# Second head's results in the other partition half, and a new order of ScalarE's copies, in a fused recurrence and expert kernel on one Trainium2 core

## What is computed

```python
for t in range(S):
    kt, vt, rt, wt = (k[:, :, t], v[:, :, t], r[:, :, t], w[:, :, t])
    cur = np.einsum('bhd,bhe->bhde', u[None] * kt, vt)
    y[:, :, t] = np.einsum('bhd,bhde->bhe', rt, state + cur)
    state = wt[:, :, :, None] * state + np.einsum('bhd,bhe->bhde', kt, vt)
```

## Time and profile before

| | |
|---|---|
| median of 3 runs | 529.81 us |
| the profiled execution, its own time | 532.97 us |
| its span | 531.0 us |
| TensorE matmul busy | 486.4 us, 92% |
| TensorE weight loads busy | 431.3 us, 81% |
| VectorE busy | 333.4 us, 63% |
| ScalarE busy | 334.9 us, 63% |

### The profile page before, as it was taken

The page is one execution under the profiler, slowest core; times in us unless marked ns, Lnnn a source line. Parts: engine busy times, 40 slices in busy tenths (PEclk is TensorE's granted clock), DMA queues, the critical chain, the costliest instruction groups (busy, mean ns, idle before and its releaser), DMA issues.

```text
span 531.0 us, 18119 instructions
## 1 busy us (share of the span) xinstructions
PE 486.4 (92%) x7516; PEld 431.3 (81%) x7516; DVE 333.4 (63%) x583; ACT 334.9 (63%) x689; POOL 13.7 (3%) x21
## 2 busy tenths in 40 slices
PE   5878999798999897888888899999999999999996
PEld 3667877687878786776434599999999999999996
DVE  8789787788888888642521575555555555555552
ACT  4788796768796977452221575656566656566653
POOL 9100000000000000000000000000000000000000
PEclk9999999899999998999999999999999999999999
DMA  8785585666363615675999220101010101010101
GB/s 166 137 175 120 121 182 105 143 126 115 65 120 67 119 33 167 204 240 156 376 394 373 88 72 1 46 1 46 0 47 1 44 0 45 0 44 1 46 0 44
DMA packets 129385, 56.19 MB, mean 106 GB/s; under 512 B 103328, under 2 KB 128928, under 8 KB 128928
## 3 DMA queue, kind: packets, MB, share of 16 engines
q1 hardware_dynamic: 126112, 54.53, 39.1%
q10 hardware_dynamic: 3200, 0.59, 0.6%
HBM read 50.38 MB, written 4.72 MB: 104 GB/s over the span
## 4 chain that ended last, share of the span: by engine, by line
PE 74%; ACT 10%; issue 6%; SPq 4%; DVE 3%; DMA 2%; ACTq 1%; DVEq 0%
PE bank L758 13%; PE bank L759 13%; PE bank L760 13%; PE lbank L482 5%; PE ybank L526 5%; PE tbank L433 5%; PE bank L748 4%; PE ybank L542 4%; ACT wide L855 4%; PE lbank L509 3%; SPq L374 2%; PE lbank L493 2%; PE ybank L463 2%; DMA w_hi<-in_moe_w_dram 2%; ACT wl L796 1%
## 5 line engine op out<-in xcount | busy, mean ns | idle before, releaser
L758 PE MATMUL bank<-wo_high,h_high 128*128 128x384 f32 x384 | 128.8, 335 | 1.4 <-DVE h_low L1251 1.2
L759 PE MATMUL bank<-wo_low,h_high 128*128 128x384 f32 x384 | 128.4, 334 | 0.0
L760 PE MATMUL bank<-wo_high,h_low 128*128 128x384 f32 x384 | 128.4, 334 | 0.0
L997 ACT ACTIVATE h_relu<-bank 128x384 f32<-128x384 f32 x128 | 62.9, 492 | 72.7 <-PE bank L748 72.4
L1249 DVE CAST h_high<-h_sq 128x384 fp32r<-128x384 f32 x128 | 46.0, 359 | 95.1 <-PE bank L760 86.3
L1085 DVE TENSOR_TENSOR rk<-rk,wl 112x768 f32<-112x768 f32 x80 | 76.5, 957 | 35.4 <-PE lbank L482 17.7
L1251 DVE TENSOR_TENSOR h_low<-h_sq,h_high 128x384 fp32r<-128x384 f32 x128 | 71.5, 558 | 4.5
L758 PEld LDWEIGHTS bank<-wo_high,h_high 128*128 128x128 f32 x384 | 72.1, 188 | 2.6 <-issue 2.2
L759 PEld LDWEIGHTS bank<-wo_low,h_high 128*128 128x128 f32 x384 | 72.1, 188 | 0.0
L760 PEld LDWEIGHTS bank<-wo_high,h_low 128*128 128x128 f32 x384 | 72.1, 188 | 0.0
L1001 ACT ACTIVATE h_sq<-h_relu 128x384 f32<-128x384 f32 x128 | 67.4, 527 | 4.1
(11 more groups left out here) (127 smaller groups left out, 543.2 us busy)
## 6 DMA issues: line engine op xcount, KB each, us to landing
w_sb<-in_moe_w_dram SPq DMA_DIRECT2D x32, 384.0 KB, 4.1
w_hi<-in_moe_w_dram SPq DMA_DIRECT2D x16, 384.0 KB, 9.2
v_tok<-in_v_dram SPq DMA_DIRECT2D x32, 144.0 KB, 3.0
w_lo<-in_moe_w_dram SPq DMA_DIRECT2D x1, 4608.0 KB, 16.5
out_dram<-o_sb SPq DMA_DIRECT2D x8, 576.0 KB, 3.0
nat<-in_r_dram SPq DMA_DIRECT2D x62, 72.0 KB, 2.5
nat<-in_k_dram SPq DMA_DIRECT2D x62, 72.0 KB, 2.7
nat<-in_w_dram SPq DMA_DIRECT2D x60, 72.0 KB, 2.6
```

The source lines that it names most:

```text
L758: nc.tensor.matmul(acc, hi, wo_high[:, fb, :], start=(fb == 0), stop=False)
L759: nc.tensor.matmul(acc, hi, wo_low[:, fb, :], start=False, stop=False)
L760: last = nc.tensor.matmul(acc, lo, wo_high[:, fb, :], start=False, stop=(fb == NF - 1))
L997: nc.scalar.activation(h_relu[fb % 2][:], h_bank[fb % 2][:, 0:GT * P], ACT.Relu).then_inc(relu_done, 1)
```

## The change

The output of `y_near` and `y_far` for head `h` of the pair goes to partition half `par ^ h`. Head 1's tokens then lie in `ybank` with the two halves exchanged, and `y_to_x` copies them back in two copies of 64 partitions, so that it has three copies instead of two. `Y_OUT` is 3 wherever `y_evac` is counted. In ScalarE's order `spread_w` of both pairs goes ahead of `y_to_x(rd - 1, 0)`, and `y_to_x(rd - 1, 1)`, which stood behind `top_level_out(rd, 0)`, goes into the next round, behind `k_out` of pair 0 (for the last but one round: between the two `k_out` behind the loop).

```diff
+    Y_OUT = 3
...
@@ after_attention, k_times_v, y_near and the wait ahead of turn_x @@
-                    pe.wait_ge(y_evac[1], 2 * rd)
+                    pe.wait_ge(y_evac[1], Y_OUT * rd)
...
+            def y_rows(par, h):
+                half = par ^ h
+                return slice(C * half, C * half + C)
+
@@ y_near @@
-                            last = nc.tensor.matmul(ybank[rows, at:at + D], aa[rd % 2][s][rows, PER * h + i, :],
+                            last = nc.tensor.matmul(ybank[y_rows(par, h), at:at + D], aa[rd % 2][s][rows, PER * h + i, :],
@@ y_far @@
-                            rows = slice(C * par, C * par + C)
-                            last = nc.tensor.matmul(ybank[rows, at:at + D], rk[rd % 3][s][a:b, 0, C * c:C * c + C],
+                            last = nc.tensor.matmul(ybank[y_rows(par, h), at:at + D], rk[rd % 3][s][a:b, 0, C * c:C * c + C],
@@ y_to_x @@
-                for h in range(2):
-                    src = ybank[:, 512 * h:512 * h + PER * D].rearrange("p (i n) -> p i n", n=D)
+                for h, a, b, to in ((0, 0, P, 0), (1, C, P, 0), (1, 0, C, C)):
+                    src = ybank[a:b, 512 * h:512 * h + PER * D].rearrange("p (i n) -> p i n", n=D)
                     at = s * PW + h * D
-                    nc.scalar.activation(X[:, :, rd, at:at + D], src, ACT.Copy).then_inc(y_evac[s], 1)
+                    nc.scalar.activation(X[to:to + b - a, :, rd, at:at + D], src, ACT.Copy).then_inc(y_evac[s], 1)
@@ ScalarE's order @@
                 if late:
                     k_out(rd - 1, 0)
+                    if rd > 1:
+                        y_to_x(rd - 2, 1)
                     widen(rd, 1, 1)
                     k_out(rd - 1, 1)
...
                 next_out(5, 1)
+                for s in range(2):
+                    spread_w(rd, s)
                 if late:
                     y_to_x(rd - 1, 0)
                 next_out(6, 1)
-                for s in range(2):
-                    spread_w(rd, s)
                 next_out(7, 2)
                 next_out(9, 1)
                 top_level_out(rd, 0)
-                if late:
-                    y_to_x(rd - 1, 1)
                 next_out(10, 2)
                 top_level_out(rd, 1)
                 if ahead:
                     widen(rd + 1, 0, 1)
-            for s in range(2):
-                k_out(ROUNDS - 1, s)
+            k_out(ROUNDS - 1, 0)
+            y_to_x(ROUNDS - 2, 1)
+            k_out(ROUNDS - 1, 1)
```

More of the change, by code:

```diff
@@ L252, in after_attention @@
             for s in range(2):
-                eng.wait_ge(y_evac[s], 2 * ROUNDS)
+                eng.wait_ge(y_evac[s], Y_OUT * ROUNDS)
         def xt_view(n):
@@ L360, in _ @@
                 for s in range(2):
-                    sp.wait_ge(y_evac[s], 2 * ROUNDS)
+                    sp.wait_ge(y_evac[s], Y_OUT * ROUNDS)
                 sp.dma_start(debug, X[:].rearrange("p a b c -> p (a b c)")).then_inc(stored[0], 16)
@@ L519, in y_near @@
                 else:
-                    pe.wait_ge(y_evac[0], 2 * (rd + 1))
+                    pe.wait_ge(y_evac[0], Y_OUT * (rd + 1))
                 for i in range(PER):
@@ L608, in _ @@
                 pe.wait_ge(top_out[s], 2 * ROUNDS)
-                pe.wait_ge(y_evac[s], 2 * (ROUNDS - 1))
+                pe.wait_ge(y_evac[s], Y_OUT * (ROUNDS - 1))
             turn_x(0, 4)
```

## The result

The changed kernel is slower: 534.48 us median (530.73 to 536.81, 20 runs) against 531.50 us (528.22 to 537.59, 20 runs) before, a ratio of 1.0063 (95% interval 1.0041 to 1.0085), some 3 us. I had forecast 3.6 us less. The page of one execution of the changed kernel, which happened to be the fastest of its 20 runs (530.73 us), shows the shares.

A forecast was written before the change was run, and what follows sets the result against it. A TensorE and a ScalarE stretch bound each round: rounds 2 to 6 -1.5, round 1 -1.1, round 7 -0.8, behind the rounds -0.2, together -3.6 us from 529.8 to 526.2 us, range 520.5 to 535.5.

The forecast's parts named there:

- Two stretches bound a round: TensorE bounds 14.1 us, level 3 of pair 0 to level 5 of pair 1; ScalarE the other 11.5 us.
- Near results at 17 ns, 0.8 us a call: `y_near` in four quarters loads weights at `L509`'s 17 ns: 0.8 us a call instead of 1.5, 0.7 us less.
- rival 1: Near results get no faster, by the row-group rule or the shared bank: +5.7 us, 535.5 us; chance 0.15.
- 0.43 us of the first call arrive: Behind the first `y_near`, level 3 of pair 1 needs `widen`, so only 0.43 of the 0.7 us passes.
- `y_far`'s order at nothing: `y_far` uses four quarters before and after; exchanging the order of two costs nothing, 0.1 us a call either way.
- `spread_w` and the third copy of pair 0 together at nothing, margin 0.2 us: `spread_w`, 1.17 us, fits ScalarE's 1.43 us idle before `y_to_x(rd-1, 0)`, paying for its third copy; else up to 0.3 us a round.
- The copies in their new place, +0.8 us: Pair 1's three `y_to_x` copies, 0.95 us mid ScalarE stretch, less 0.15 us of wait, lengthen it by 0.8 (0.45 to 0.95).
- The sum over rounds 2 to 6, -0.3 each: TensorE stretch -1.1 us plus ScalarE stretch +0.8 us gives -0.3 us a round, -1.5 us in all.
- Round 1, -1.1: The first round has the faster near results but no moved copies yet: -1.1 us.
- The last round -0.8 and what lies behind it -0.2: Round 7: -1.3 on TensorE, +0.5 for copies; behind: two `y_near` calls -1.4, `turn_x` +0.6, last copies +0.3, `x_out` +0.3.
- Rival 4: ScalarE's copies hold more than they last, some 0.3 us a round: -1.8 us in all, 528 us; chance 0.1.
- The base: The sum is taken from the median of three runs, 529.8 us, not from the profiled execution's 532.97 us.

The follow-up runs named there:

- VectorE's copies: Changed kernel with VectorE copying head 1, ScalarE only head 0, `y_to_x` of pair 1 back in its own round; ratio 1.0024 to the kernel before.
- the four quiet profiles: Kernel before and changed kernel, each run twice with all w1 loads behind the recurrence: 559.98 and 560.96 us before, 564.53 and 564.02 us changed.

## Why the prediction was wrong

Point by point, in its own order:

- *Two stretches bound a round.* Right. Every version moved as the stretch in which it changed something, and the chain of the changed kernel runs through the same pieces. (That more than half of TensorE's busy time lies behind 300 us was a misreading: it is 225 of 486 us. Nothing hung on it.)
- *Near results at 17 ns, 0.8 us a call.* Right: 17 ns, and the shared bank did not matter. So rival 1 has fallen: the order of row halves stayed the same, and going round four quarters instead of two nearly halved the spacing. The rule of the Trainium skill that loads overlap matmuls only of another row group ("TensorE: Matmul & The Clock Gate", Part 3, What overlaps and what doesn't), by which there was to be no gain, is not borne out by this trace.
- *0.43 us of the first call arrive.* It was 0.33, for the 0.15 us between `widen` and the matmul behind it.
- *`y_far`'s order at nothing.* Right, 22 to 23 ns.
- *`spread_w` and the third copy of pair 0 together at nothing, margin 0.2 us.* **This step failed.** Two things in it were wrong. The move of `spread_w` cannot pay for input copy 6: on ScalarE's list copy 6 stands directly behind `y_to_x(rd - 1, 0)` before the change as after it, and `spread_w` stood behind copy 6. And the three copies take 1.27 us, not 0.95. So copy 6 came 0.69 us later behind the first copy, turn 8 waited, and a round lost 0.36 us of the near gain; -1.1 us became -0.66. With copy 6 first, turn 8 no longer waited.
- *The copies in their new place, +0.8 us.* 0.86, within its bounds, but in part by luck: the copies cost 1.17 us where I had 0.95, and 0.3 us came back where I had 0.15.
- *The sum over rounds 2 to 6, -0.3 each.* Follows from the above: +0.2 each, +1.0 in all in place of -1.5.
- *Round 1, -1.1.* Its TensorE stretch, from level 3 of pair 0 to the end of level 5 of pair 1, has no issue gap in the four quiet profiles. It takes 14.07 and 14.10 us before, and 13.44 and 13.91 changed: -0.6 and -0.2.
- *The last round -0.8 and what lies behind it -0.2.* Wrong by more than the rounds. From the first `y_near` of the last round to that behind the rounds, where I had -0.8 and +0.6 for the first `turn_x`, the quiet pairs have +1.3 and +1.4 us. The waits that I had priced came out about as forecast (0.8 us ahead at the last `turn_k`, then 0.74 us of waiting where I had 0.6). What I had no term for are issue gaps and the clock, which took the rest. From that `y_near` to the expert part I had -0.8, and it is -0.1 us in both pairs: the two calls give 1.3 us, but `x_out` behind three copies takes 0.7 of it back and the wait for the last copies 0.56 (1.44 us in place of 0.88), where I had 0.3 for each. That is again the length of three copies.
- *Rival 4* (copies that hold more than they last) named the right part, but I gave it 0.1 and a size that still left a gain.
- *The base.* I started from 529.8 us, the median of three runs; that of 20 is 531.5. This is 1.7 of the 8.3 us between forecast and measurement.
- *The range* (520.5 to 535.5 us) holds the median, and within 2% is right; the sign is not.

What stays open: of the 3 us, rounds 2 to 6 account for 1.0, and the end of the recurrence for some 1.4 in the quiet pairs. Every version with the exchange loses more than its rounds say: with VectorE's copies 4.5 us of shorter rounds end in 1 us more time. That a TensorE with less to do runs into more issue gaps and a lower clock agrees with the sums of gaps in the mean, less clearly with the mean clocks, and no run here turns either on and off by itself. The one interval that ends below 1 (0.9928 to 0.9999) belongs to a kernel that leaves the halves exchanged, and is one of fourteen; no version that computes the right result is shown faster than the kernel before.

## What to carry to other kernels

When an engine that alternates with another on the chain is made faster, count the full price on the other one first: here 0.7 us won on TensorE twice a round was paid with two more copies on ScalarE and a bank handed back later. When one piece is moved away to pay for another, read the list of the order: only what stood behind the moved piece comes earlier. Take the length of an added instruction from a row with the same form and the same neighbour, and treat a margin of 0.2 us as none. And a round that is 0.6 us shorter in the trace need not show in the time: look at the last round, the issue gaps and the clock of several profiles before counting it.

## What the runs showed of the hardware

The three copies do not overlap as the two of before do. Two copies of 128 partitions start 0.31 us apart and take 0.71 us; the three of now start 0.44 and 0.43 us apart and take 1.27 us, although the last two have half as many partitions. The timeline puts the first of them at 148.96, and the chain of the changed kernel, which takes it up at 149.07, shows the starts of the others:

```profile
149.07 0.30 ACT xs L876
149.38 0.03 issue
149.40 0.41 ACT xs L876
149.81 0.02 issue
149.83 0.40 ACT xs L876
```

What keeps them apart (the number of partitions, the other half, or the bank that the last two share) no run here tells.

Issue gaps of TensorE stand at fixed places of the instruction stream. Counted in matmul records from the start (the first is record 0), those of the kernel before between 40 us and the end of the last `y_near` stand right ahead of records 712, 1586, 1711, 1962, 2087, 2461, 2838, 4963, 5215 and 5341: each time within 2 records of a multiple of 125 behind the one before. Other profiles have gaps at more places of the same grid, and how long a gap is varies: 0.44 us before and 0.98 us changed at record 2461, which is the 22nd of a `y_near`. The page of the kernel before lists a queue of instructions beside those of the data:

```profile
q8 instruction: 57, 0.93, 0.8%
```

Each of its packets has 16,384 bytes, and almost every stretch of 125 records (125 weight loads and 125 matmuls, some 4 us) has one. The traces hold the packets' times. In the 20 profiles there are 207 issue gaps in this part, and in all of them TensorE goes on 1.06 to 1.74 us after a packet of q8 has ended (nine in ten: 1.25 to 1.57 us). In the longest gap of the kernel before (2.14 us, until 100.65 us) the packet ran from 98.33 to 99.32 us, and the one ahead of it had ended at 92.93. So the gaps are waits for late packets of instructions. Why a packet is late, and whether a faster TensorE alone makes more of them late, no run here tells.
